# A second layer-1 square per chunk computed in halves, its full square on GpSimd, and the next chunk's input split moved

## The reference

```python
# attention: q (12288 tokens x 128), kv (384 x 32 x 128) averaged over 4x4 blocks -> 768 keys
kv_flat = kv_pool.reshape(B, -1, C) @ w_sr ; k = v = kv_flat
a = softmax(q @ k.T / sqrt(C)) ; x = a @ v
# layer 1
h = x @ w_in ; r = np.maximum(h, 0.0) ; x = (r * r) @ w_out          # 128 -> 2048 -> 128
# layer 2
h = x @ w_in ; h2 = h * h ; h3 = h2 * h
P = a[0] + a[1]*h + a[2]*h2 + a[3]*h3
Q = 1.0 + |b[0]|*|h| + |b[1]|*h2
out = (P / (Q + 1e-6)) @ w_out                                          # 128 -> 2048 -> 128
```

## Time and profile before

| | |
|---|---|
| time, median of 3 runs | 1517.66 us (1517.64 to 1517.86) |
| the profiled execution's own time | 1517.89 us |
| its span, first to last instruction | 1515.9 us |
| attention, up to the first layer-1 matmul | 293.0 us |
| PE busy, 320 to 1400 us | 1079.54 of 1080 us |
| DVE busy there | 1069.91 us |
| ACT busy there | 1057.51 us |
| POOL busy there | 1010.19 us |
| PE's granted clock | full in all slices |

### The profile page before, as it was taken

The page is one execution under the profiler, slowest core; times in us unless marked ns, Lnnn a source line. Parts: engine busy times, 40 slices in busy tenths (PEclk is TensorE's granted clock), DMA queues, the critical chain, the costliest instruction groups (busy, mean ns, idle before and its releaser), DMA issues.

```text
span 1515.9 us, 20584 instructions
## 1 busy us (share of the span) xinstructions
PE 1483.7 (98%) x5576; PEld 991.1 (65%) x5576; DVE 1445.2 (95%) x2549; ACT 1378.8 (91%) x2672; POOL 1248.3 (82%) x1225
## 2 busy tenths in 40 slices
PE   5999999999999999999999999999999999999988
PEld 4999999765666666666666666666666666666655
DVE  7888888889999999999999999999999999999998
ACT  3777777689999999999999999999999999999997
POOL 4544445359999999999999999999999999999897
PEclk9999999999999999999999999999999999999999
DMA  6200001000000000000000000000000000000000
GB/s 224 84 21 28 21 27 43 1 1 1 8 8 8 1 8 8 8 8 1 7 8 8 0 8 8 8 1 8 7 8 1 8 8 8 8 1 8 8 8 7
DMA packets 11518, 24.21 MB, mean 16 GB/s; under 512 B 1440, under 2 KB 2336, under 8 KB 11168
## 3 DMA queue, kind: packets, MB, share of 16 engines
q1 hardware_dynamic: 11424, 23.14, 4.5%
HBM read 16.85 MB, written 6.29 MB: 15 GB/s over the span
## 4 chain that ended last, share of the span: by engine, by line
PE 88%; DVE 5%; ACT 2%; POOL 2%; issue 1%; DMA 1%; SPq 0%; POOLq 0%; ACTq 0%; DVEq 0%
PE psum L937 19%; PE psum L974 18%; PE psum L801 11%; PE psum L800 11%; PE psum L802 11%; PE psum L889 6%; PE psum L852 6%; PE psum L874 4%; DVE tb L727 1%; DVE tb L736 1%; DVE tb L753 1%; DVE g1h L713 1%; DVE psum L741 1%; POOL tb L410 1%; DMA X<-kvT 1%
## 5 line engine op out<-in xcount | busy, mean ns | idle before, releaser
L412 POOL TENSOR_TENSOR wb<-wb,ub 128x512 f32<-128x512 f32 x384 | 496.4, 1293 | 29.4
L937 PE MATMUL psum<-tb,wout 128*128 128x512 f32 x736 | 375.8, 592 | 2.5 <-DVE tb L785 2.3
L974 PE MATMUL psum<-g,wout 128*128 128x512 f32 x690 | 352.4, 592 | 0.2 <-ACT x2f L528 0.2
L404 POOL TENSOR_SCALAR wb<-ub,babs 128x512 f32<-128x512 f32 x384 | 296.0, 771 | 35.5 <-ACT ub L550 30.3
L800 PE MATMUL psum<-x2h,win2h 128*128 128x512 f32 x384 | 283.3, 738 | 2.6 <-POOL x2l L397 2.5
L727 DVE SCALAR_TENSOR_TENSOR tb<-tb,ca,psum 128x512 f32<-128x512 f32 x364 | 267.8, 736 | 4.6 <-ACT psum L584 4.5
L736 DVE SCALAR_TENSOR_TENSOR tb<-tb,ca,psum 128x512 f32<-128x512 f32 x365 | 269.6, 739 | 0.0
L551 ACT ACTIVATE tb<-psum,ca 128x512 f32<-128x512 f32 x384 | 267.1, 696 | 0.0
L550 ACT ACTIVATE ub<-psum 128x512 f32<-128x512 f32 x384 | 233.0, 607 | 23.5 <-PE psum L802 23.5
L568 ACT ACTIVATE lnb<-wb 128x512 f32<-128x512 f32 x384 | 248.3, 647 | 5.2 <-POOL wb L412 4.8
L753 DVE SCALAR_TENSOR_TENSOR tb<-psum,tb 128x512 f32<-128x512 f32 x364 | 248.1, 682 | 2.6
(11 more groups left out here) (109 smaller groups left out, 2506.6 us busy)
## 6 DMA issues: line engine op xcount, KB each, us to landing
qraw<-qT SPq DMA_DIRECT2D x23, 256.0 KB, 2.6
outT<-osb SPq DMA_DIRECT2D x23, 256.0 KB, 2.0
X<-kvT SPq DMA_DIRECT2D x15, 384.0 KB, 7.7
wraw<-w_in SPq DMA_DIRECT2D x2, 1024.0 KB, 8.3
X<-kvT SPq DMA_DIRECT2D x2, 192.0 KB, 10.5
outT<-osb SPq DMA_DIRECT2D x2, 128.0 KB, 1.8
qraw<-qT SPq DMA_DIRECT2D x1, 192.0 KB, 10.2
wsr<-w_sr SPq DMA_DIRECT2D x1, 64.0 KB, 1.8
```

The costliest lines, as they stand in the source:

```text
L404: nc.gpsimd.tensor_scalar(w, u, babs[:, 1:2], babs[:, 0:1], ALU.mult, ALU.add).then_inc(v_rdy, 1)
L412: nc.gpsimd.tensor_tensor(w, w, u, ALU.mult).then_inc(w_rdy, 1)
L937: mm(ACC2, wout2[:, f, :], tb[:, t % T_RING, :], start=(f == 0), stop=(f == NF - 1))\
L974: mm(ACC1, wout1[:, f, :], g1[:, t % G_RING, :], start=(f == 0), stop=(f == NF - 1))\
```

## The change

`SPLIT_COLS` gets a second column, 5, so blocks of column 5 are halved in chunks 1 to 23 as those of column 13 are. For each, ACT makes a `g1h` at step 6, POOL makes a `g1l` at the end of step 5, after the square that it does in either kernel, and PE's `out1` at step 7 is three matmuls. `x1_high` moves from the head of POOL's step 5 to the head of step 6, and `x1_low` to the head of step 8 (chunks 1 to 22). Line numbers above 391 are one higher in the changed kernel.

```diff
-        SPLIT_COLS = (13,)
+        SPLIT_COLS = (5, 13)
 ...
             for s in range(STEPS):
-                if s % NF == 5 and 1 <= s // NF < NCH - 1:
+                if s % NF == 6 and 1 <= s // NF < NCH - 1:
                     x1_high(s // NF + 1)
+                if s % NF == 8 and 1 <= s // NF < NCH - 1:
                     x1_low(s // NF + 1)
```

## The result

| | before | after |
|---|---|---|
| median | 1517.80 us (6 runs) | 1527.14 us (6 runs, 1526.97 to 1527.65) |
| span of the profiled execution | 1515.9 us | 1525.1 us |
| first `in1` of chunk 1 to that of chunk 2 | 43.01 us | 44.30 us |
| the same for chunks 4 to 23, median | 49.65 us | 49.98 us |

The ratio is 1.0061, 95% interval 1.0049 to 1.0074: 9.3 us slower, where 1527 had been forecast.

A forecast was written before the change was run, and what follows sets the result against it. PE, 98% busy, was taken as the bound. A late chain adds 0.44 us a chunk: 22 x 0.44 = +9.7 on 1517.89 gives 1527.6, 0.2 less for the median, taken as 1527 us; range 1518 to 1531.5.

The forecast's parts named there:

- The handover: Layer-2 input from POOL's `x2l` to PE's `in2` at step 3: no slack, PE waits 0.59 us per chunk.
- The chain: From `in2` at step 3 over ACT and POOL to the next one: 50.09 us, where PE alone needs 49.50.
- The sum: 22 chunks at +0.44 us give +9.7 us; chunk 23 gives back 0.16 at most; 1527 us forecast.
- PE's gain: Steps around column 5's `out1`, 23 blocks: 3.113 to 2.957 us, -0.156 each, -3.6 us if nothing is late.
- added square: `g1h` on ACT at step 6: 0.53 us, hidden because ACT waits for PE at even steps.
- DVE: Hides its own lateness: 1.5 us of room against Exp's about 1 us; its pace is below 50.09 a chunk.
- A: Faster: POOL's holes take the new work and PE's saving is whole, 1514.1 us; chance 0.10.
- B: No change: lateness halved, PE waits about 0.16 us a chunk, which eats the saving, 1517.7 us; chance 0.06.
- C: Slower: late Exp makes DVE late by over 1.5 us, PE waits for layer-2 results mid-chunk, 1534 us; chance 0.08.

The follow-up runs named there:

- the two orders at the end: Against the kernel before: columns 5 (from chunk 2), 11 halved, x1 at steps 1, 3, 1515.16 us; columns 5 (from chunk 2), 13, x1 at 3, 7, 1514.27 us.

## Why the prediction was right

**The handover.** The claim that Abs of step 1, if late, stops PE at step 3 in every chunk was right. Its size in the trace is 0.48 where 0.59 was forecast. In this kernel `x2l` is also the only exit by which PE is stopped. What was incomplete is that other exits stand ready behind it (`x2f`, `osb`), which cost PE time once `x2l` comes sooner, as the run with the shorter `x2l` showed.

**The chain.** Its pieces, measured in the changed kernel around one chunk:

| | forecast | measured |
|---|---|---|
| `in2` of step 3 to `v` of step 5 | 7.82 | 7.84 (1069.49 to 1077.33) |
| on to `v` of step 13 | 25.61 | 25.51 (1077.33 to 1102.84) |
| on to `v` of step 1 | 12.04 | 12.08 (1102.84 to 1114.92) |
| on to `x2l` | 3.12 | 3.12 (1114.92 to 1118.04) |
| on to PE's `in2` | 1.50 | 1.44 (1118.04 to 1119.48) |
| sum | 50.09 | 49.99 |

1069.49 and 1119.48 are PE's first slots of `in2`, by the starts of its second matmul (1069.72 and 1119.71) less 0.235. Of the 16 handovers, 3 go this way in the profile's chain and 13 over ACT, as said; the forecast had only the way over PE.

The 0.10 in the second row comes mostly from POOL's small terms: `x1h` follows the `g1l` after 1.22 instead of 1.26 and takes 0.60 instead of 0.63, `x1l` starts 1.00 after the square instead of 1.03, L411 0.74 after `v` instead of 0.78. These rows show it:

```profile
1030.64 1.28 POOL L424 TENSOR_TENSOR g1l<-g,g1h 128x512 fp32r<-128x512 f32 x1
1031.86 0.61 POOL L348 CAST x1h<-X 128x512 fp32r<-128x512 f32 x1
1032.46 0.78 POOL L405 TENSOR_SCALAR wb<-ub,babs 128x512 f32<-128x512 f32 x1
...
1036.70 1.03 POOL L419 TENSOR_TENSOR g<-r 128x512 f32<-128x512 f32 x1
1037.70 1.29 POOL L353 TENSOR_TENSOR x1l<-X,x1h 128x512 fp32r<-128x512 f32 x1
...
1044.22 0.77 POOL L405 TENSOR_SCALAR wb<-ub,babs 128x512 f32<-128x512 f32 x1
1044.95 1.29 POOL L411 TENSOR_TENSOR tb<-tb,hcb 128x512 f32<-128x512 f32 x1
```

Ln waits for `w` in steps 7, 9 and 11, as forecast: it starts 0.83, 1.41 and 0.80 after the Identity ahead of it, which is 0.57 where nothing is waited for. Together it waits 1.3 us in this chunk, where over 1 had been forecast.

**The sum.** The time was hit more closely than its terms deserve, and part of that is luck. A steady chunk costs 0.33 more instead of 0.44: chunks 3 to 22, with a single one of 50.30, cost 6.7 us, and 22 laps at this price 7.3 instead of 9.7. A term was missing, the start of layer 2, and with it chunk 1 costs 1.3 us and chunk 2 only 0.2. Chunk 23 with the run-out adds 0.9, where the prediction had it give back 0.16 at most, and the attention part 0.1. That makes the 9.2 by which the span grew. A price per chunk that was 0.11 too high and terms that weren't in the sum cancel.

**PE's gain** of 0.156 a chunk is real: the kernel without the added `g1l`, and the two orders at the end, run at 49.49 to 49.50. **ACT's** added square was priced at nothing; at most 0.06 a chunk hangs on it. **DVE** was left off the path: it has a wait for Exp in the changed kernel's steady chunks (4.3 us in 16), but none of PE's there names DVE. It was wrong for the start, for the kernel with x1 at step 5, and above all for the one with the shorter `x2l`, whose round of waits runs over DVE from step 11 to step 4.

**The rivals.** A, that POOL's holes take the work, is what happens in another order of the same work, and its price was right: 1514.1 worked out for 23 blocks, 1514.27 measured for 22 with x1 at steps 3 and 7. B and C didn't occur.

**Open** is why the steady chunk is 49.98 in the changed kernel and 49.92 where only chunk 1 differs. It is not the place of the buffers. The traces differ in where the chain passes the handover: over ACT in 13 of 16 chunks of the changed kernel, over `x2l` and PE in 14 of 16 of the other. Why is not shown.

## What to carry to other kernels

Idle time of an engine that others wait for is not a sum to be spent: ask at which steps it lies, and follow the work from there to the next handover that has no slack. Here the same work cost 9 us in one order and nothing that can be told from zero in another; with one block less in halves, a third order gained 3.4. When a cut at the handover gains less than the stop that it removes, look for a second round of waits: here it was only 0.06 us a chunk shorter than the first. A just-in-time handover shows in the profile as a weight load that waits, with a matmul behind it that doesn't.

## What was not expected of the hardware

On POOL the distance from one instruction to the next depends a little on what follows: `x1_high` starts 1.22 us after a `g1l`, `v` 1.26 after one; `x1_low` 1.00 after a square, `v` 1.02. And where PE's `in2` had to wait, its first matmul had its slot 1.44 us after `x2l` began, by the start of the second at 1119.71 less 0.235, or 0.1 after its weight load started at 1119.37, though the trace has that load as 0.19 long. The prediction had left open whether a matmul waits for its whole load. If this one takes its 0.235 like the others, it didn't.
